# Attention with values in plain fp32, each half of the tokens in 64 columns of TensorE, and sums of exponentials made apart

## What is computed

```
q_bits = (q @ proj > 0); k_bits = (k @ proj > 0)          # proj: 64 x 6
mask   = bucket(q_bits)[:, None] == bucket(k_bits)[None, :]
scores = where(mask, q @ k.T / 8, -1e9)
scores = scores - max(scores)
attn   = exp(scores);  attn = attn / (sum(attn) + 1e-9)
x      = attn @ v                                         # 16 heads, then 1536 x 512
x      = prelu(x @ w_in1, alpha) @ w_out1
x      = rational(x @ w_in2; a, b) @ w_out2
```

## Time and profile before

| | us |
|---|---|
| runs before, median of three | 801.62 (801.29 to 804.07) |
| the profiled execution: own time, span of the core | 804.17, 802.3 |
| of the span, the attention (to the last `empty_rows`) | 271.4 |
| PE busy over the span | 789.8 (98%) |
| DVE, ACT, POOL busy over the span | 560.8, 425.6, 287.7 |

### The profile page before, as it was taken

The page is one execution under the profiler, slowest core; times in us unless marked ns, Lnnn a source line. Parts: engine busy times, 40 slices in busy tenths (PEclk is TensorE's granted clock), DMA queues, the critical chain, the costliest instruction groups (busy, mean ns, idle before and its releaser), DMA issues.

```text
span 802.3 us, 11341 instructions
## 1 busy us (share of the span) xinstructions
PE 789.8 (98%) x3628; PEld 640.4 (80%) x3628; DVE 560.8 (70%) x877; ACT 425.6 (53%) x653; POOL 287.7 (36%) x364
## 2 busy tenths in 40 slices
PE   8989999999999999999999999999999999999998
PEld 5677887887888888888888888888888888888886
DVE  7868888888885654335333543379888988888886
ACT  7657788788787510112101201157667666676673
POOL 7556665666673779400000077782000000000000
PEclk9989999999999999999999999999999999999999
DMA  4555666765764143100000033320000100000001
GB/s 126 144 140 151 169 166 157 180 165 152 183 159 110 55 142 121 46 1 1 0 1 14 0 91 94 95 89 14 1 0 1 53 2 0 1 19 35 1 1 52
DMA packets 34078, 58.80 MB, mean 73 GB/s; under 512 B 9836, under 2 KB 13652, under 8 KB 34036
## 3 DMA queue, kind: packets, MB, share of 16 engines
q1 hardware_dynamic: 33748, 58.22, 26.5%
q10 hardware_dynamic: 288, 0.04, 0.0%
HBM read 29.54 MB, written 3.19 MB: 41 GB/s over the span
## 4 chain that ended last, share of the span: by engine, by line
PE 91%; DMA 2%; SPq 2%; POOL 2%; ACT 1%; DVE 1%; issue 1%; POOLq 0%; PEldq 0%; DVEq 0%
PE ps_h L1283 33%; PE acc L1315 33%; PE ps_o L572 11%; PE ps_a L487 4%; PE ps_s L542 3%; PE ps_s L547 3%; PE ps_a L484 2%; DMA stage<-in_w_out 1%; DMA raw<-in_qk 1%; PE ps_o L583 1%; DMA k<-pen 0%; PE ps_a L500 0%; POOL w_early_in_lo L883 0%; POOL w_early_out_lo L883 0%; PE ps_s L590 0%
## 5 line engine op out<-in xcount | busy, mean ns | idle before, releaser
L1348 ACT ACTIVATE g_hi<-num 128x512 fp32r<-128x512 f32 x96 | 59.8, 624 | 205.3 <-PE acc L1315 201.6
L1418 DVE TENSOR_TENSOR g_lo<-num,g_hi 128x512 fp32r<-128x512 f32 x96 | 72.4, 754 | 78.8 <-ACT g_hi L1348 78.3
L986 DVE TENSOR_REDUCE row_max<-ps_a 128x1 f32<-128x384 f32 x180 | 91.9, 552 | 25.4 <-PE ps_a L487 23.9
L681 ACT ACTIVATE ps_s<-ps_s 128x768 f32<-128x768 f32 x96 | 76.6, 798 | 48.4 <-PE ps_s L547 48.2
L1016 DVE TENSOR_TENSOR p_lo<-ps_s,p_hi 128x768 fp32r<-128x768 f32 x96 | 90.9, 948 | 15.1 <-ACT p_hi L688 13.2
L688 ACT ACTIVATE p_hi<-ps_s 128x768 fp32r<-128x768 f32 x96 | 78.0, 812 | 3.7
L1283 PE MATMUL ps_h<-x_hi,w_late_in_lo 128*128 128x512 f32 x288 | 78.8, 394 | 0.0
L1283 PE MATMUL ps_h<-x_lo,w_late_in_hi 128*128 128x512 f32 x288 | 78.8, 394 | 0.0
L1283 PE MATMUL ps_h<-x_hi,w_late_in_hi 128*128 128x512 f32 x288 | 78.8, 394 | 0.0
L1356 ACT ACTIVATE den_q<-ps_h,abs_b 128x512 f32<-128x512 f32 x48 | 33.1, 689 | 83.4 <-PE ps_h L1283 79.4
L1426 DVE TENSOR_SCALAR num<-ps_h,alpha_sb 128x512 f32<-128x512 f32 x48 | 36.0, 750 | 54.5 <-PE ps_h L1283 54.2
(11 more groups left out here) (173 smaller groups left out, 1727.6 us busy)
## 6 DMA issues: line engine op xcount, KB each, us to landing
stage<-in_w_in SPq DMA_DIRECT2D x26, 256.0 KB, 2.7
stage<-in_w_out SPq DMA_DIRECT2D x26, 256.0 KB, 2.7
raw<-in_qk SPq DMA_DIRECT2D x15, 384.0 KB, 3.2
q<-hi SPq DMA_DIRECT2D x30, 192.0 KB
k<-hi SPq DMA_DIRECT2D x30, 192.0 KB
v_raw<-in_v SPq DMA_DIRECT2D x16, 192.0 KB, 3.0
work<-rden_scratch SPq DMA_DIRECT2D x16, 192.0 KB, 3.4
out<-y SPq DMA_DIRECT2D x12, 256.0 KB, 2.6
```

The lines of the kernel that those rows point to most:

```text
L681: nc.scalar.activation(p32, p32, ACT.Exp, scale=float(D) ** -0.5).then_inc(s_exp, 1)
L986: dve.tensor_reduce(row_max[slot][:, i, c:c + 1], ps_a[:, i, 0:HALF], AX.X, ALU.max).then_inc(s_a_free, 1)
L1348: nc.scalar.activation(g_hi[f % 2][:], num[f % 4][:], ACT.Copy).then_inc(s_ghi, 1)
L1418: dve.tensor_tensor(g_lo[f % 2][:], num[f % 4][:], g_hi[f % 2][:], ALU.subtract).then_inc(s_glo, 1)
```

## The change

- `values` takes the unrounded `v_use` and the unrounded exponentials `p[c]`, both fp32, in two matmuls a chunk. Each half of the queries has 64 columns of PE and 64 partitions of one bank of `ps_o`: half 0 in 0 to 63, half 1 in 64 to 127. Rounding copies of the exponentials and of `v`, and `p_lo` and `v_lo`, are gone.
- The sums: DVE adds the chunks two by two (`add`), three results a head, and `sums` multiplies them with 32 columns of ones, in plain fp32, each quarter of the queries in 32 columns of its own: 12 matmuls of 192 columns, in the next head. ACT copies the quarters out, DVE takes the reciprocals of 128x192 elements, and SP stores four rows of 192, once a head instead of once a pair. `turn_den` is gone.
- The second half of a `bits` use goes to columns 32 to 55.
- The work goes by groups of two chunks (one in head 0): scores and uses of the one, scores and uses of the other, then `values` of both, then the uses behind. `empty_rows` and `sums` of the head before stand ahead of the first `values`.
- The lists of uses are new: `a` of chunk 0 stands right behind the first scores of a head, `bits` behind the second, the turn behind the first group's `values`.
- ACT: the one exponential goes straight from `ps_s` to `p[c]`. `split_qk` is moved from ahead of the exponential of the next head's chunk 0 to behind it.

```diff
 def uses_of(left, u, first_head, second_head):
...
-                begin = [("bits", 3, 0)] if bits else [("a", 2, 0)] if more else []
-                return [(begin, [("a", 2, 0)] if bits else []),
-                        ([("m", 1, 0)], [("a", 2, 1)] if more else []),
-                        ([], [("a", 2, 2)] if more else []),
-                        ([], [("a", 2, 3)] if more else []),
-                        ([], [("a", 2, 4)] if more else []),
-                        ([], [("a", 2, 5)] if more else [])]
+                return [([("a", 2, 0)] if more else [], [("m", 1, 0)]),
+                        ([("bits", 3, 0)] if bits else [], []),
+                        ([("a", 2, 1)] if more else [], [("a", 2, 3)] if more else []),
+                        ([("a", 2, 2)] if more else [], []),
+                        ([("a", 2, 4)] if more else [], [("a", 2, 5)] if more else []),
+                        ([], [])]
...
 SP, in a head
-                        if u == 0 and not (isinstance(j, int) and j == 0):
-                            store_rows(sp, j - 1)
+                        if not (isinstance(h, int) and h == 0):
+                            store_rows(sp, 1 - u, j - 1 + u, den_row[1 - u][:])
                         if left > 1 or (left == 1 and u == 0):
                             fill_a(1 - u, j + 1 + u)
...
-                        if left or u == 0:
-                            turn_den(sp, u, j, h)
...
 PE
-                            m = pe.matmul(ps_a[0:4 * BITS, i, 0:HALF], pj[:, 0:PJ_APART], raw[slot][:, half], start=True, stop=True)
+                            m = pe.matmul(ps_a[BIT_AT[place]:BIT_AT[place] + 4 * BITS, i, 0:HALF], pj[:, 0:PJ_APART],
+                                          raw[slot][:, half], start=True, stop=True)
...
 def values(slot, h, c, t):
-                    for k, (w, p) in enumerate(((v_hi, p_hi), (v_lo, p_hi), (v_hi, p_lo))):
-                        for i in range(2):
-                            m = pe.matmul(ps_o[0:WIDE[slot], i, 0:HALF], w[slot][:, c, 0:WIDE[slot]],
-                                          p[r][:, i * HALF:(i + 1) * HALF], start=(c == 0 and k == 0), stop=False)
-                    m.then_inc(s_pv, 1)
+                    for i in range(2):
+                        m = pe.matmul(ps_o[OUT[i], 0, 0:HALF], v_use[slot][:, c], p[c][:, i * HALF:(i + 1) * HALF],
+                                      start=False, stop=(c == KC - 1))
+                    m.then_inc(s_head if c == KC - 1 else s_pv, 1)
...
+                def sums(h):
+                    pe.wait_ge(s_add, KC // 2 * (h + 1))
+                    if due(h):
+                        pe.wait_ge(s_sums, h)
+                    for n in range(KC // 2):
+                        for i in range(4):
+                            rows = slice(i * QUARTER_ROWS, (i + 1) * QUARTER_ROWS)
+                            m = pe.matmul(ps_o[rows, 1, 0:QUARTER], ones[:], p_sum[n][:, i * QUARTER:(i + 1) * QUARTER],
+                                          start=(n == 0), stop=(n == KC // 2 - 1))
+                    m.then_inc(s_summed, 1)
...
+                        for begin in range(0, KC, group):
+                            for c in range(begin, begin + group):
+                                t = KC * h + c
+                                if c + 2 < KC:
+                                    scores(u, j, c + 2, t + 2)
+                                elif not (final and u == 1):
+                                    scores(1 - u, j + u, c + 2 - KC, t + 2)
+                                for kind, g, cc in steps[c][0]:
...
+                            if begin == 0:
                                 empty_rows(u, h)
+                                if not first:
+                                    sums(h - 1)
+                            for c in range(begin, begin + group):
+                                values(u, h, c, KC * h + c)
+                            for c in range(begin, begin + group):
+                                for kind, g, cc in steps[c][1]:
...
 ACT, in a head
                         for c in range(KC):
                             t = KC * h + c
+                            if c == (3 if first and u == 0 else 2) and not last:
+                                stat_rows(1 - u, j + u)
+                            if c + 2 < KC:
+                                exponential(c + 2, h, t + 2)
+                            elif not last:
+                                exponential(c + 2 - KC, h + 1, t + 2)
+                            if c == 1 and not (first and u == 0):
+                                sums_of(1 - u, j - 1 + u, h - 1)
+                            if c == 3 and not last:
+                                copy_v(1 - u, j + u)
                             if c == 4 and (left > 1 or (left == 1 and u == 0)):
                                 split_qk(1 - u, j + 1 + u)
-                            if c + 2 < KC or not (final and u == 1):
-                                exp32((c + 2) % KC, t + 2)
-                            if c + 2 < KC or not (final and u == 1):
-                                exp_high((c + 2) % KC, t + 2)
...
 DVE, in a head, after the uses of a group
+                                if side == 0 and (begin + group) % 2 == 0:
+                                    add((begin + group) // 2 - 1, h)
+                            if begin == 2 and not (first and u == 0):
+                                reciprocal(dve, 1 - u, h - 1, den_row[1 - u][:])
...
+                def add(n, h):
+                    dve.wait_ge(s_exp, KC * h + 2 * n + 2)
+                    if due(h):
+                        dve.wait_ge(s_summed, h)
+                    dve.tensor_tensor(p_sum[n][:], p[2 * n][:], p[2 * n + 1][:], ALU.add).then_inc(s_add, 1)
```

More of the change, by code:

```diff
@@ L85, in build_program @@
         x32, rden_bc = work[:, 0:S], work[:, S:2 * S]
[L86 to L92, removed]
+        guard = sb_in(outer, "guard", [P, 1])
+        s_sums = sem("s_sums")
+        s_rden = [sem(f"s_rden{u}") for u in range(2)]
+        s_rst = [sem(f"s_rst{u}") for u in range(2)]
         s_rbc = sem("s_rbc")
@@ L102, in build_program, with store_rows, reciprocal @@
         s_w = sem("s_w")
[L105 to L109, removed]
+        def store_rows(sp, u, j, row):
+            sp.wait_ge(s_rden[u], j + 1)
+            dst = rden_dram[bass.ds(j, 1)].rearrange("a u (n t) -> (a u n) t", n=4)[4 * u:4 * u + 4]
+            sp.dma_start(dst, row[0:P:QUARTER_ROWS]).then_inc(s_rst[u], 16)
         def spread(sp, j):
-            sp.wait_ge(s_rst, 16 * (j + 1))
             for u in range(2):
+                sp.wait_ge(s_rst[u], 16 * (j + 1))
+            for u in (1, 0):
                 src = rden_dram[bass.ds(j, 1)].rearrange("a u s -> (a u) s")[u:u + 1]
                 sp.dma_start(rden_bc[D * u:D * u + D], src.broadcast_to([D, S])).then_inc(s_rbc, 16)
[L118 to L121, removed]
+        def reciprocal(dve, u, h, row):
+            dve.wait_ge(s_sums, h + 1)
+            dve.reciprocal(row, row).then_inc(s_rden[u], 1)
         def x_high(act, j):
@@ L150, in build_program @@
             v_raw = [sb(f"v_raw{u}", [P, KC, D]) for u in range(2)]
-            v_hi = [sb(f"v_hi{u}", [P, KC, (D + 2, P)[u]], F32R) for u in range(2)]
-            v_lo = [sb(f"v_lo{u}", [P, KC, (D + 2, P)[u]], F32R) for u in range(2)]
+            v_use = [sb(f"v_use{u}", [P, KC, D]) for u in range(2)]
+            idle = sb("idle", [P, HALF], F32R)
+            ones = sb("ones", [P, QUARTER_ROWS])
             v_three = sb("v_three", [P, 3, D])
@@ L292, in use_counts @@
                     left = min(2, PAIRS - 1 - h // 2)
-                    for before, after in uses_of(left, h % 2, h == 0, h == 1):
-                        for kind, g, c in before + after:
-                            n += 2
-                            done[kind, h + g, c] = n
+                    steps, group = uses_of(left, h % 2, h == 0, h == 1), group_of(h == 0)
+                    for first in range(0, KC, group):
+                        for side in range(2):
+                            for step in steps[first:first + group]:
+                                for kind, g, c in step[side]:
+                                    n += 2
+                                    done[kind, h + g, c] = n
                 return done, pair_start
@@ L940, in pair @@
                             normalise(j - 1)
-                        if not (final and u == 1):
-                            split_v(1 - u, h + 1)
                         if left > 1 or (left == 1 and u == 0):
@@ L1532, in mlp_vector @@
                 step(0, 0, 0, False, None)
-                reciprocals(dve, PAIRS - 1)
+                reciprocal(dve, 1, HEADS - 1, rden_bc[:, 0:QUARTER])
                 def tile(layer, t, final):
```

284 lines of the change are left out of this document (119 added, 165 removed).

## The result

The changed kernel takes 841.57 us (median of four runs, 837.77 to 848.33) against 802.81 for the kernel before in the same comparison: 1.0491 times as long, interval 1.0445 to 1.0538. The forecast was 846. The profiled execution of after took 848.33, its core's span is 846.3, and its mean granted clock is 0.969. The other three runs had 0.976 (845.16), 0.987 (837.98) and 0.987 (837.77), so the spread of ten microseconds goes with the clock: the longer the run, the lower its mean clock. Against the profiled execution of before (804.17) it is +44.2; forecast were +44.4.

The account below looks back on a forecast made before the run. PE's issue bounds the kernel until a wait is longer; the `ka` filling wait then sets 18.94 a head. Eleven periods of 3.70 give +40.7, with the ends +44.4: 848.6 profiled, 846 against the median, range 810 to 890.

Parts of the forecast that it names:

- eight instructions of values: PE's fp32 values products of a two-chunk group: five times 0.32, 1.61 a group, between 1.29 and 2.58 as ends.
- sums, 24 instructions: PE's products of 192 columns for the sums: 13 steps of 0.16, 2.08; serial 3.86, overlapped in fours 0.96.
- `a` to the end of the next head's first scores: PE's own work from `a` of chunk 0 to the end of the next head's chunk 0 scores, 12.59.
- from there to the use of the next `a`: After those scores: 0.16, exponential 0.80, rounding 0.84, 0.10 between, filling of `qa` and `ka` 4.45; together 6.35.
- PE's wait for `ka`: PE idle ahead of the first `a` of each head until the filling DMA ends, about 2.0.
- a head at the full clock: Period of a middle head set by the filling chain: 12.59 + 6.35 = 18.94, against 15.24 before.
- all the rest: Heads outside the repeated middle periods: head 0 +1.0, head 1 −2.8, head 13 +1.0, head 14 +0.5, head 15 +4.0.
- If only neighbours in different columns overlap: PE's narrow fp32 products overlap only between one product's second instruction and the next's first; this forecast of 846 had chance 0.38.
- the first rival: PE's products in different columns overlap wholly, with the wait for `ka` remaining: period +1.94, total 817; chance 0.27.
- a tie at 14.6 of the head: Filling released equally late by ACT's rounding and by SP's store waiting for DVE's reciprocal, both at 14.6.
- the clock falls: PE's clock drops to half after the waits, up to 3.4 in each of 12 heads, +41, total 887; chance 0.10.
- not slower: Products overlap wholly and the filling comes in time: period 15.2 by PE's own work, total 793; chance 0.16.

Follow-up runs that it names:

- e8: e2 with POOL's `x_low` of the pair before moved from odd heads to behind `row_stats` of even ones; 800.93 against 802.13, ratio 0.9976.
- e4: Changed kernel with both halves' values products of chunks 0 to 4 in the same columns, output wrong; 881.99 against 803.86, ratio 1.0965.
- e7: Changed kernel with a group's values products reordered, half 0 of both chunks, then half 1 of both; 844.6, ratio 1.0491 without one execution.
- e2: Changed kernel with ACT's rounding back ahead of the exponential and SP's store of the reciprocals behind the filling; 809.33 against 803.86, ratio 1.0074.
- e5: Changed kernel with only ACT's rounding put back ahead of the exponential, the store staying ahead of the filling; 855.37 against 802.13, ratio 1.0653.
- e6: Changed kernel with only SP's store of the reciprocals moved behind the filling, the rounding staying behind the exponential; 838.12, ratio 1.0436.
- e9: Changed kernel with 22 dummy products in PE's wait for `ka` (heads 2 to 11) and POOL's `x_low` one head later; 836.67 against 802.51, ratio 1.043.
- e10: Changed kernel with only POOL's `x_low` moved one head later; one execution 838.39, three 854.04 to 857.19, no ratio given.
- e1: Changed kernel with 22 unused rounded products on PE ahead of the wait for `ka` in heads 2 to 11; 840.77, ratio 1.0448.
- e11: e8's kernel once more, twelve runs in five rounds, against the kernel before; 801.26 against 802.51, ratio 0.9985.

## Why the prediction was right, and where not

The time came out 4 us from the forecast, but that is luck: several steps were off, in both directions.

| step | forecast | measured |
|---|---|---|
| eight instructions of values | 1.61 | 1.29 |
| sums, 24 instructions | 2.08 | 1.11 |
| `a` to the end of the next head's first scores | 12.59 | 11.09 |
| from there to the use of the next `a` | 6.35 | 7.06 to 7.54 |
| PE's wait for `ka` | 2.0 | 2.7 to 2.9 |
| a head at the full clock | 18.94 | 18.15 to 18.63 |
| half the clock in heads 2 to 12 | none | 47.8 us, cost 14.2 |
| heads 2 to 12, ten periods, against before (152.67) | +37.0 | +45.2 |
| all the rest | +7.4 | −1.0 |

**Values and sums: the term was mis-sized.** "If only neighbours in different columns overlap" was the step that failed. With it fell the sentence that PE's work alone needs 17.26 a head: in e8, where hardly a wait is left, a head with all that work takes 15.15 to 15.54, so that nearly all of the loss is idle time and clock, not PE's work. Products in different columns overlap wholly (after, e4, e7), the price of the first rival. The bits use of before, from which I took the step of 0.32, could not tell this apart, since its two instructions were in the same columns. The Trainium skill, page "TensorEngine Tiling (Array Packing)", section "Key Properties", has it right, that different tiles work in parallel. Its page "TensorE: Matmul & The Clock Gate", Part 3, says that matmuls start in program order; e7's records differ from that, half 1's first product having started ahead of half 0's second, and the measurement decides.

**The wait sets the period: right, and the reason for the loss.** PE idles ahead of the first `a` of each head, released by a DMA of `ka`, 31.4 us in twelve times, eleven of them 2.46 to 2.86. e2 shows the cause by removal: 38.8 us over the kernel before become 5.5. The forecast called ACT's path and SP's path a tie at 14.6 of the head; e5 and e6 show that they are nearly one, with SP's the longer by 0.56 (18.15 against e6's 17.59): the reciprocal took 1.34 instead of the 1.2 estimated, and between its end and the filling lie 0.9 to 1.0 with the store's issue, where I had 0.5. This is most of 7.06 − 6.35.

**The clock: the rival came in part.** I gave "the clock falls" 0.10 and a price of up to 41. It fell in nine of the heads 2 to 12 (not in 2 and 5), for longest in the late ones, and cost 14.2 of the profiled execution; the runs of 837.8, at a mean clock of 0.987 against 0.969, lost less. e9 against e10 shows that it belongs to the idle time: the 22 products in it are all that differs, and the mean clock was 0.989 to 0.997 in four runs with them and 0.953 to 0.987 in four without. And the narrow products alone don't bring the clock down: e8 has every one of them, and 1.00 from 45 to 290. What decides in which heads it falls is not settled: with e5's idle time of 2.75 it fell in every head from 3 to 12, with after's of 2.67 to 2.86 for 3.4 us in four of heads 2 to 7 and for 6.8 in all of 8 to 12; in e6 it fell with idle times of 2.26, in e2 once with one of 1.09, and one execution of e10 had far less of it than the three others. Where it falls in each head, the head takes 20.3 to 20.6 in after, e5, e7 and e10 alike, which the work at full clock (18.15 or 18.63) doesn't give.

**POOL beside DVE: not foreseen.** I priced the addition by L1016 at 0.95. That row has one operand in PSUM and never took more than 0.96 in 96 times; the addition has both in SBUF and took up to 2.40 in after, 2.44 in e2 and 3.81 in e1. The Trainium skill, page "SBUF — State Buffer", section "SBUF: two separate sides", says that an operation of DVE with two inputs in SBUF and one of GpSimd that reads SBUF lock each other out for a whole instruction. e2's rows agree: the addition ended 0.82 behind POOL's 1.82. So does e8, where POOL's operation is moved away and the addition takes 0.96 again. In the head of after shown above it costs 0.48 (7.54 − 7.06), in e2 about 1.65 every second head (16.81 against 15.16).

**Head 1 and the ends.** The forecast had +7.4 for them and −1.0 was measured. From head 0's to head 1's empty rows it took 22.20 with 3.4 us at half the clock, which I had ruled out. The overlap that I priced too low probably brings the rest back, since heads 0, 14 and 15 carry many narrow products and no wait for `ka`; no run divides this further.

**So the forecast hit by offsetting errors.** Full overlap with the wait was the better model: 17.18 by the rival, 0.26 more of PE's work and 0.71 more of the chain make 18.15. A head on average: 18.94 forecast, −1.50 for the work up to the scores, +0.71 for the chain, +1.42 for the clock and +0.21 for waits behind the additions (e9's 18.36 − 18.15) make 19.78; measured were 19.79. Of the +44.2, 31.0 is the wait's in ten heads (183.63 − 152.67), with these waits in it, 14.2 the clock's, and −1.0 the rest. So the ten heads lost 8.2 more than forecast and all the rest 8.4 less, and no reason joins the two. The rival "not slower" exists, too: e8 has its period, 15.40 on average over the ten heads against its 15.2 and before's 15.27, once both chains are out of the way and POOL's operation as well; the 793 that went with it was not reached (e11, 801.26).

## What to carry to other kernels

When a change moves the place of a use earlier and the step that feeds it later, add up the chain from the event that releases the step to the use, on each queue, and count every path into the same DMA: shortening one of two nearly equal ones gave no clear gain or a longer time, shortening both 33 us. Narrow products in different columns could be costed here as those of one set of columns; but where PE's work isn't the bound, what they save becomes idle time, and here idle times of 2.3 to 2.9 in each period cost the clock as well. A sum of two tensors in SBUF should be kept away from GpSimd's long operations, or be priced with their full length on top.

## What the runs showed of the hardware

- Plain fp32 products in two sets of 64 columns start in pairs 6 to 7 ns apart and cost 0.32 a pair of instructions of 384 columns; four sets of 32 cost 24 instructions of 192 columns 1.11 with the change of width. A product could start ahead of one that stood before it in the program but used the other columns (e7).
- A reciprocal of 128x192 fp32 elements took 1.34 us on VectorE, one of 128x12 0.22: about 6.2 ns an element.
- The same program ran middle heads at 18.2 and 18.6 with the clock at 1.00 and at 20.5 with 6.8 us at 0.50 in each head (after), and stayed in the second for many heads in a row once there (after, e5, e10).
- Dummy products that filled 2.74 of an idle time of about 2.9 kept the clock at 1.00 in heads 2 to 11; behind the unfilled 2.68 of head 12 it fell for 3.4 (e9). The ten heads took 18.36 on average, and 20.41 without the products (e10).
- An addition of two 128x768 fp32 tensors in SBUF takes 0.95 on VectorE alone; begun during a GpSimd operation it ended 0.82 behind that one (e2).
